# Folding the gate weights inside block 0, with reordered loads and scatters, in a fused attention and expert kernel

## What is computed

```
for t in range(S):
    m_new = np.maximum(f_gate[:, :, t] + m, i_gate[:, :, t])
    f_stab = np.exp(f_gate[:, :, t] + m - m_new); i_stab = np.exp(i_gate[:, :, t] - m_new); m = m_new
    C = f_stab * C + i_stab * outer(v_t, k_t);   n = f_stab * n + i_stab * k_t
    y[:, :, t] = sigmoid(o_gate_t) * (C @ q_t) / max(|n . q_t|, 1)
h = x @ w_in                                   # 3072 x 320 by 320 x 2048
g = where(h >= 1, h, where(h <= -1, 0, (h + 1)**2 / 4))
x2 = g @ w_out                                 # 2048 x 320
logits = x2 @ w_gate;  e = argmax(logits);  gate = softmax(logits)[e]
out[token] = gate * (relu(x2 @ w1[e]) @ w2[e]) # 8 experts, 320 x 1024 and 1024 x 320
```

## Time and profile before

| | us |
|---|---|
| median of 3 runs | 816.65 |
| lowest, highest | 814.5, 816.67 |
| profiled execution | 823.59 |
| its span, first to last instruction | 821.4 |
| PE busy | 768.7 (94%) |
| DVE, ACT, POOL busy | 595.2, 422.9, 318.5 |

### The profile page before, as it was taken

The page is one execution under the profiler, slowest core; times in us unless marked ns, Lnnn a source line. Parts: engine busy times, 40 slices in busy tenths (PEclk is TensorE's granted clock), DMA queues, the critical chain, the costliest instruction groups (busy, mean ns, idle before and its releaser), DMA issues. The chain is left out here.

```text
span 821.4 us, 17203 instructions
## 1 busy us (share of the span) xinstructions
PE 768.7 (94%) x5765; PEld 746.8 (91%) x5765; DVE 595.2 (72%) x1009; ACT 422.9 (51%) x649; POOL 318.5 (39%) x297
## 2 busy tenths in 40 slices
PE   2789999999999999999999999988979899999994
PEld 1788999999999999999999999988979899999994
DVE  4653768787878787878878788648677857676751
ACT  3022545454545454545454545663466766666761
POOL 3341543545343434454544444541434141313111
PEclk9999999999999999999999999998989999999998
DMA  6962222222222222222323210566647554338400
GB/s 198 308 174 75 75 93 76 90 75 90 74 90 74 90 74 93 81 95 85 94 87 92 83 40 1 174 160 171 236 145 228 205 198 158 121 94 266 148 7 5
DMA packets 41458, 97.05 MB, mean 118 GB/s; under 512 B 6936, under 2 KB 24482, under 8 KB 39755
## 3 DMA queue, kind: packets, MB, share of 16 engines
q1 hardware_dynamic: 37498, 87.46, 34.0%
q0 software_dynamic: 3920, 9.08, 3.6%
HBM read 105.63 MB, written 9.33 MB: 140 GB/s over the span
## 5 line engine op out<-in xcount | busy, mean ns | idle before, releaser
L552 POOL TENSOR_TENSOR g_t<-u_t,r_t 128x512 f32<-128x512 f32 x96 | 135.7, 1414 | 257.0 <-ACT u_t L702 256.9
L697 ACT ACTIVATE r_t<-bank,neg 128x512 f32<-128x512 f32 x96 | 66.0, 688 | 189.9 <-PE bank L1446 189.9
L1458 PE MATMUL bank<-wo_h,g_h 128*128 128x328 f32 x384 | 127.2, 331 | 0.0
L1033 DVE TENSOR_SCALAR u_t<-bank 128x512 f32<-128x512 f32 x96 | 66.1, 688 | 76.2 <-ACT r_t L697 49.2
L1458 PE MATMUL bank<-wo_h,g_l 128*128 128x328 f32 x384 | 120.2, 313 | 0.0
L1458 PE MATMUL bank<-wo_l,g_h 128*128 128x328 f32 x384 | 120.1, 313 | 0.0
L634 POOL DMA_INDIRECT out_x<-ob,idx_tok x31 | 37.4, 1208 | 153.8 <-ACT ob L772 149.5
L702 ACT ACTIVATE u_t<-u_t,half 128x512 f32<-128x512 f32 x96 | 69.5, 724 | 39.6 <-DVE u_t L1033 38.0
L969 DVE TENSOR_TENSOR_SCAN W<-W,cst 128x512 f32<-128x512 f32 x48 | 83.2, 1737 | 5.0 <-DMA W<-decays 5.0
L1579 PE MATMUL bank<-w_h,h_h 128*128 128x320 f32 x248 | 79.4, 320 | 7.4 <-DVE w_l L1097 6.3
L1446 PE MATMUL bank<-xT_h,wi_h 128*128 (+1 forms) x384 | 79.5, 289 | 1.6 <-issue 1.6
(11 more groups left out here) (234 smaller groups left out, 1949.9 us busy)
## 6 DMA issues: line engine op xcount, KB each, us to landing
raw<-in_w SPq DMA_DIRECT2D x10, 1280.0 KB
W<-decays SPq DMA_DIRECT2D x24, 512.0 KB, 5.0
raw2n<-in_w SPq DMA_DIRECT2D x9, 1280.0 KB
raw<-in_w SPq DMA_DIRECT2D x10, 1024.0 KB
raw1n<-in_w SPq DMA_DIRECT2D x9, 1024.0 KB
raw<-in_w SPq DMA_DIRECT2D x20, 256.0 KB
raw1n<-in_w SPq DMA_DIRECT2D x18, 256.0 KB
qG<-in_q SPq DMA_DIRECT2D x24, 180.0 KB
```

Of the source, the lines that this page charges most:

```text
L552: pool.tensor_tensor(g_t[p % 2][:, :], u_t[p % 2][:, :], r_t[p % 2][:, :], ALU.add).then_inc(sm["g_done"], 1)
L697: act.activation(r_t[p % 2][:, :], bank_h[p % 2][:, :], ACT.Relu, bias=neg1[:, 0:1]).then_inc(sm["r_done"], 1)
L1033: dve.tensor_scalar(u_t[p % 2][:, :], bank_h[p % 2][:, :], 1.0, -1.0, ALU.min, ALU.max).then_inc(sm["u_done"], 1)
L1458: mm = pe.matmul(bank_acc[tt][:, 0:DL], l[p % 4][:, c], r[:, f, :], start=f == 0 and a == 0, stop=f == NT1 - 1 and a == 2)
```

## The change

- `FOLDS` lists four folds of four row tiles, after steps 0, 3, 5 and 6 of block 0. `fold(n)` leaves `ahead` and stands in PE's `body` behind `second` of that step. Fold n from the second on waits until VectorE has taken the columns of fold n - 1 from `bank_r`.
- `logit_columns(n)` on VectorE, one step later and ahead of `clamp`, both rounds and subtracts 32 columns. `hi_logits` and `lo_logits` go. `second` of block 0 waits for the columns that it multiplies.
- `keep_awake(5)` is new: five bf16 matmuls of 512 columns, all ones, into `bank_acc[0]`, which `second` starts anew later. It stands in `ahead` in front of `turn_x(t, 1)` and again behind it. `to_state(t, 1)` moves ahead of the first.
- SP: the fill and the zero row go right behind unit 1; w_out half 0 ahead of wT half 0; half 1 of w_in next; unit 0 of block 1 is loaded ahead of wT half 1 and w_out half 1. ScalarE waits for fill and zero row at the end of `ahead`.
- GpSimd: in `ahead` both parts of w_in's half 1 move behind unit 1's values and state, the second into step 1 of block 0. In the last block `to_table` of the block before moves from behind step 7 to behind `gated` of step 6.
- ScalarE: `x_high(t, 1)` ahead of `hi_dense(1)`. VectorE: `weigh(t, 1, 1)` ahead of `x_low(t, 0)`.
- Joint: `y_low(4)` ahead of `h_low(3, 3)`; y(6) ahead of w1(6) on ScalarE and VectorE; `second2(2)` is cut behind tile 4 instead of 5.

The names in the rows below: xs, qT, Vp and C are attention operands, wg and wT those of the fold, a number ahead of the line is the place in the engine's list.

The diff, with its less telling lines left out:

```diff
+FOLDS = ((0, 0, 4), (3, 4, 8), (5, 8, 12), (6, 12, 16))
 NU = B * CH
...
             def body(t, prev, att):
-                if att:
+                if not prev:
+                    load_unit(t + 1, 1)
+                elif att:
                     ahead(t + 1)
...
                 load_unit(t, 1)
+                sp.wait_ge(sm["prep"], 3)
+                sp.dma_start(slots_dram.rearrange("(p a) c -> p (a c)", p=P), fill[:, :]).then_inc(sm["prefill"], 16)
+                sp.dma_start(x2_dram[N:N + 1, :], zrow[0:1, :]).then_inc(sm["zrow"], 16)
                 sp.dma_start(wg[:, 0:2, :], w_gate[0:2 * P, :].rearrange("(c p) e -> p c e", p=P)).then_inc(sm["wg_in"], 16)
                 sp.dma_start(wg[0:TAIL, 2, :], w_gate[2 * P:DM, :]).then_inc(sm["wg_in"], 16)
                 sp.dma_start(wg[64:64 + TAIL, 2, :], w_gate[2 * P:DM, :]).then_inc(sm["wg_in"], 16)
+                load_dense_second(0)
                 load_turned(0)
+                load_dense(1)
+                load_unit(t + 1, 0)
                 load_turned(1)
-                load_dense_second(0)
-                load_dense(1)
                 load_dense_second(1)
-                sp.wait_ge(sm["prep"], 3)
-                sp.dma_start(slots_dram.rearrange("(p a) c -> p (a c)", p=P), fill[:, :]).then_inc(sm["prefill"], 16)
-                sp.dma_start(x2_dram[N:N + 1, :], zrow[0:1, :]).then_inc(sm["zrow"], 16)
...
                 values(t, 1)
-                lo_dense(1, 0)
                 values_end(t, 1)
                 decay_state(t, 1)
-                lo_dense(1, 1)
+                lo_dense(1, 0)
...
                     gated(t, p)
+                    if not prev and p == 1:
+                        lo_dense(1, 1)
                     if not att and p == 1:
...
                         gather(p - 4)
-                if prev:
+                    if not att and p == 6:
+                        to_table(t - 1)
+                if prev and att:
                     to_table(t - 1)
...
-            def hi_logits():
-                act.wait_ge(sm["wp_ready"], 2)
-                act.activation(wo_h[:, :, DM:DL], bank_r[:, 0:NT1 * E].rearrange("p (t e) -> p t e", e=E), ACT.Copy).then_inc(sm["wp_hi"], 1)
             act.wait_ge(sm["gate_lf"], 1)
...
                 hi_second(0)
+                x_high(t, 1)
                 hi_dense(1)
-                x_high(t, 1)
-                hi_logits()
+                act.wait_ge(sm["prefill"], 16)
+                act.wait_ge(sm["zrow"], 16)
...
             h_high(5, 3)
+            y_high(6)
             w1_high(6, 0)
             w1_high(6, 1)
             for s in range(5, NS):
                 if KINDS[s] == "H":
                     h_plain(s, 0)
                     h_plain(s, 1)
-                if s + 1 < NS:
+                if 6 < s + 1 < NS:
                     y_high(s + 1)
...
-            def lo_logits():
-                dve.wait_ge(sm["wp_hi"], 1)
-                dve.tensor_tensor(wo_l[:, :, DM:DL], bank_r[:, 0:NT1 * E].rearrange("p (t e) -> p t e", e=E),
-                                  wo_h[:, :, DM:DL].bitcast(F32), ALU.subtract).then_inc(sm["wp_lo"], 1)
+            def logit_columns(n):
+                rows = slice(FOLDS[n][1], FOLDS[n][2])
+                folded = bank_r[:, FOLDS[n][1] * E:FOLDS[n][2] * E].rearrange("p (t e) -> p t e", e=E)
+                dve.wait_ge(sm["wp_ready"], n + 1)
+                dve.tensor_copy(wo_h[:, rows, DM:DL], folded).then_inc(sm["wp_hi"], 1)
+                dve.wait_ge(sm["wp_hi"], n + 1)
+                dve.tensor_tensor(wo_l[:, rows, DM:DL], folded, wo_h[:, rows, DM:DL].bitcast(F32), ALU.subtract).then_inc(sm["wp_lo"], 1)
...
                 weigh(t, 1, 0)
+                weigh(t, 1, 1)
                 x_low(t, 0)
-                weigh(t, 1, 1)
                 lo_dense(0)
                 outputs(t, 1)
                 new_state(t, 1)
                 x_low(t, 1)
-                lo_logits()
...
                         early_experts(t)
+                    for n, (at, lo, hi) in enumerate(FOLDS):
+                        if not prev and p == at + 1:
+                            logit_columns(n)
                     clamp(t, p)
...
             w1_low(4, 0)
+            y_low(4)
             h_low(3, 3)
-            y_low(4)
             w1_low(4, 1)
...
             h_low(5, 3)
+            y_low(6)
             w1_low(6, 0)
             w1_low(6, 1)
             for s in range(5, NS):
-                if s + 1 < NS:
+                if 6 < s + 1 < NS:
                     y_low(s + 1)
...
                     pe.wait_ge(sm["x2_ready"], t * 2 + 1)
+                if isinstance(t, int) and t == 0:
+                    pe.wait_ge(sm["wo_lo"], p // 4 + 1)
+                    pe.wait_ge(sm["wp_lo"], min(n + 1 for n, (at, lo, hi) in enumerate(FOLDS) if hi >= 2 * p + 2))
                 pe.wait_ge(sm["gl_done"], n + 3)
...
-            def fold(half):
-                if half == 0:
-                    pe.wait_ge(sm["wg_in"], 48)
-                pe.wait_ge(wT_in[half], 32)
-                for i in range(NT2):
-                    f = NT2 * half + i
+            def fold(n):
+                at, lo, hi = FOLDS[n]
+                if n >= 1:
+                    pe.wait_ge(sm["wp_lo"], n)
+                for f in range(lo, hi):
+                    half, i = f // NT2, f % NT2
+                    if i == 0:
+                        pe.wait_ge(sm["wg_in"], 48)
+                        pe.wait_ge(wT_in[half], 32)
                     cols, tcols = slice(f * P, f * P + P), slice(i * P, i * P + P)
...
                 mm.then_inc(sm["wp_ready"], 1)
+            def keep_awake(n):
+                for _ in range(n):
+                    pe.matmul(bank_acc[0][:, :], ones_b[:, :], ones_b[:, :].unsqueeze(1).to_broadcast([P, 4, P]), start=True, stop=True)
...
                 to_state(t, 0)
-                fold(0)
                 attention(t, 1, 0)
                 turn_x(t, 0)
                 attention(t, 1, 2)
-                fold(1)
-                attention(t, 1, 3)
+                to_state(t, 1)
+                keep_awake(5)
+                turn_x(t, 1)
+                keep_awake(5)
             def body(t, prev, att):
                 for p in range(NP1):
                     if not prev and p % 4 == 0:
                         pe.wait_ge(sm["wi_lo"], p // 2 + 2)
-                    if not prev and p % 4 == 2:
-                        pe.wait_ge(sm["wo_lo"], p // 4 + 1)
-                    if not prev and p == 2:
-                        pe.wait_ge(sm["wp_lo"], 1)
                     first(t, p)
...
                         second(t - 1, NP1 - 2 + p)
+                    for n, (at, lo, hi) in enumerate(FOLDS):
+                        if not prev and p == at:
+                            fold(n)
+                    if not prev and p == NP1 - 1:
+                        pe.wait_ge(sm["wp_lo"], len(FOLDS))
                     if not att and p == 0:
...
                 turn_y(3)
-                second2(2, range(3, 6))
+                second2(2, range(3, 5))
                 first2(3)
                 turn_y(4)
-                second2(2, range(6, NT2))
+                second2(2, range(5, NT2))
                 first2(4)
```

## The result

| | before | changed |
|---|---|---|
| median of 13 runs, us | 817.2 | 811.25 |
| lowest, highest | 814.5, 823.08 | 805.96, 819.31 |
| profiled execution, its span | 823.59, 821.4 | 815.08, 813.3 |
| PE busy | 768.7 | 765.1 |

The ratio is 0.992 (95% interval 0.9895 to 0.9946). The change made the kernel faster, by 0.8% or 6 us, but 797 was forecast and 808 was the end of the range. The profiled executions lie 8.5 us apart.

A forecast was written before the change was run, and what follows sets the result against it. TensorE, busy nearly all the time, was taken as the bound. Head (-19.8 + 11.8 - 3.4 + 0.5 = -10.9 us) and joint (-8.9) gave -19.8, subtracted from the plain median 816.65: 797 us, range 790 to 808.

The forecast's parts named there:

- The start of block 0: Head: with the folds out of the attention chain, block 0 starts at 49.3 instead of 69.07, 19.8 us earlier.
- The folds: Block 0: all 16 fold tiles come back there and cost 11.8 us at 2.4 GHz, bounds 11.5 and 23.
- The clock: Start of block 0: PE rises to 2.4 GHz during first(0, 0) and stays there, 3.4 us gained.
- The first rival: Block 0: the clock falls at folds (three falls, about 8 us, 805) or rises late (803); chance 0.28.
- The wait at `turn_x`: Block 0: VectorE behind GpSimd's subtraction of w_in's second half lengthens PE's 1.17 us wait by 0 to 2.0, taken as 0.5.
- The joint: Between dense and routed blocks and in waits after it: earlier scatters and reordered y save 8.9 us.
- -6.1 and -2.6: Joint: PE's idle 6.12 us before 557.83 goes, and with it 5.3 us at half speed, worth half.
- the 0.4 for y(4): Joint: y_low(4) moved ahead and a second2(2) tile moved behind first2(3) save 0.4 us, 0 to 1.1.
- I subtract the same: Plain runs, median 816.65, were taken to gain as many us as the profiled execution, giving 797.
- The slower rival: Block 0 at 1.2 GHz throughout: 29 us slower in front, 20 in all, 837; chance 0.04.
- More in front: Head: the dummies raise the clock before first(0, 0) and the wait at turn_x shrinks, 794; chance 0.06.
- The joint gives back: Joint: the removed idling becomes another wait and half of the 8.9 us is lost, 801; chance 0.12.

The follow-up runs named there:

- e7_table_alone: The kernel before with one edit: the scatters of block 10's slots after step 6 on GpSimd instead of step 7; 811.52 us, ratio 0.9931.
- e2_head_alone: The changed kernel with the joint's edits undone, so only the head's edits remain; 813.45 us, ratio 1.002 to the kernel before.

## Why the prediction was wrong, step by step

**The start of block 0, right.** -19.8 forecast, -21.7 measured. The chain of attention was freed as worked out. The dummies cost nothing instead of 1.4 us: PE reached them at 43.11 instead of 44.1, and most of them ran at the full clock.

**The folds, a little too cheap.** I scaled by intra's matmuls and got 11.8 us for 16 tiles. A row of four took 3.43 us without a fall (50.50 to 53.93), 13.7 in all: +1.9. Before it was 11.25 us for eight tiles at 1.2 GHz, so full clock brings the fold to 0.61 of its time, not to 0.51.

**The clock, the step that failed.** The sentence was: "I expect the rise during first(0, 0), which costs 1.2 of half speed: 3.4 us gained", and with it "the forecast needs 2.4 GHz throughout". The rise did come, even sooner. But PE then lost 13.6 us in 27.3 us at half speed, where before it lost 4.6. So the term was +9.0 and not -3.4, counting half of the time at half speed as lost. The first rival had the mechanism, at 0.28, and mis-sized it: three falls, 8 us, 805. There were five stretches, of 3.4, 3.4, 6.8, 10.2 and 3.4 us, and the longer two held through whole products of `first`, scores, intra and `second` before the clock came back. The evidence against my forecast stood in my own rows: 11 us of folding without a gap had not raised the clock in the head. I took it as a sign about raising and not about holding. The Trainium skill, "TensorE: Matmul & The Clock Gate", section "HAM oscillation — how this bites in real kernels", lays falls of the clock to waits that leave TensorE idle; here the fall at 68.0 and the one in the kernel with a third of the fold agree (1.96 and 3.06 us of waiting), but those behind the folds come without any gap, so for them the trace says otherwise.

**The wait at `turn_x`, right.** It grew from 1.17 us, and 0.22 at the intra ahead of it, to 1.96: +0.6, 0.5 was forecast. VectorE beside GpSimd is how:

```profile
65.27 0.29 DVE L1001 SCALAR_TENSOR_TENSOR den<-num 128x8 f32<-128x8 f32 x1
65.59 1.20 DVE L1003 TENSOR_SCALAR den<-den 128x8 f32<-128x8 f32 x1
...
65.49 1.27 POOL L556 TENSOR_TENSOR g_t<-u_t,r_t 128x512 f32<-128x512 f32 x1
```

An operation on 8 columns that takes 0.17 us elsewhere took 1.20 and ended 0.03 us behind GpSimd's. It was the g of step 1, though, not the subtraction of w_in that I had named; that one (2.38 us from 61.21) stood ahead of g on GpSimd with two operations between, all without a gap.

Head: -21.7 + 13.7 + 9.0 + 0.6 makes +1.6; the timelines say +0.7 (110.68 to 111.41). Most of the 0.9 left over comes of counting half: no matmul here takes twice as long at 1.2 GHz. Those of `second` start every 0.27 us instead of every 0.15, the pairs of `first` every 0.42 instead of 0.24, so a microsecond at half speed loses about 0.44. By that the clock's term is an estimated +7.9 and the sum +0.5. The forecast was -10.9.

**The joint, right in the profile, too large in the runs.** -8.9 forecast, -8.9 between the two traces: the waits of PE from 540 on add up to 10.4 us instead of 14.8, and 11.3 us of busy half speed went, 5.6 us; about 1 us of small differences goes the other way. Of the terms, -6.1 and -2.6 are as written, the scatters ahead of g cost 0.9 (0.2 forecast, bound 1.5), the 0.4 for y(4) came as 1.4 (2.81 to 2.55, and 1.10 gone), though e7_table_alone has as much without y(4), y(6) gave nothing, as costed, and the second fall, at 601.63, which I had left in, went too in this trace. In plain runs it was 5.8 us. The step that failed here is "I subtract the same": the kernel before loses less clock in most plain runs than in the profiled ones (median 0.991 against 0.988).

Together from 797: +12.4 for the clock, +1.9 for the folds, -1.9 for the start, +3 for the joint, 812.4 against 811.25 measured. That it comes so close is in part luck: the terms of the head are those of one pair of executions, 6.4 and 3.8 us above the medians, and the head's plain runs spread over 8 us.

**Rivals.** The slower rival named its point, nine tenths of block 0 at half speed; it was 27.3 of 64.1 us. That point was worked out wrongly: by the prediction's own terms (-19.8 + 11.8 - 4.6 + 0.5 - 8.9 = -21.0) the kernel turns slower once the clock loses 21 us, some 42 us at half speed, which is about six tenths of a block 0 that long. "More in front" was true of the rise and worth 1 us. "The joint gives back" lost 3 us, by the clocks of the plain runs more to a gain that they didn't have to give than to a new wait.

## What to carry to other kernels

Before a filler of small matmuls is moved into a dense stretch of TensorE, ask what it does to the clock: look in the trace for a place where the same matmuls already ran, and what the granted clock did there. Put such fillers in singly between wide matmuls, not in rows: block 0 lasted 57 to 65 us with the 16 tiles in rows of four (three traces) and 51 to 52 with them one by one (two traces). And read the mean granted clock of every run before a profiled execution is taken as the typical one.

## What was not expected of the hardware

- TensorE without a gap fell to 1.2 GHz: inside or right behind 11 of 12 rows of four fold tiles (3.4 us of 128x128 weight loads with 8 columns each), at both rows of three, behind none of the four rows of two that ran at full clock, and once behind two tiles that followed a third tile and the scores. With the tiles spread, block 0 stayed at 1.00 in two traces and fell once, for 3.4 us, in a third.
- Once down it stayed down for 3.4, 6.8, 10.2 and up to 20.5 us with TensorE busy all the time, when attention and fold rows were mixed into the steps. What brings it back up is not shown.
- With ten dummies of 512 columns ahead of block 0 the clock was up before it in every trace (0.47 or 0.48 us for the first pair of firsts); without them that pair took 0.76, and 16 us of block 0 passed at 1.2 GHz.
- A wait of 2.40 us at the same place ahead of `first2(6)` let the clock fall in it or 1.2 us behind it in two traces (e7_table_alone, e2_head_alone) and not in two others (the kernel before, twice).
- 64 columns instead of 8 in the fold matmuls did not keep the clock up (13.6 us at half speed in block 0).
